# The odd 64 rows of a 320-row contraction as pairs of half-row matmuls into two PSUM banks

## What is computed

```python
def _moe_ref(x, w_gate, w_val, w_out, rms_g):      # d_model 320, d_ff 1536
    rms = np.sqrt(np.mean(x * x, axis=-1, keepdims=True) + 1e-06)
    xn = x / rms * rms_g
    g = xn @ w_gate
    silu = g * (1.0 / (1.0 + np.exp(-g)))
    return (silu * (xn @ w_val) @ w_out)

def _moe2_ref(x, w_in, w_out):                     # d_model 320, d_ff 2048
    h = x @ w_in
    return (np.maximum(0.01 * h, h) @ w_out)
```

## Time and profile before

| | |
|---|---|
| median of 3 runs | 477.48 us (476.37 to 477.69) |
| the profiled execution, first to last instruction (its span) | 473.8 us |
| TensorE busy | 95% of the span |
| VectorE, ScalarE, GpSimd busy | 56%, 38%, 22% |

### The profile page before, as it was taken

The page is one execution under the profiler, slowest core; times in us unless marked ns, Lnnn a source line. Parts: engine busy times, 40 slices in busy tenths (PEclk is TensorE's granted clock), DMA queues, the critical chain, the costliest instruction groups (busy, mean ns, idle before and its releaser), DMA issues.

```text
span 473.8 us, 7144 instructions
## 1 busy us (share of the span) xinstructions
PE 452.0 (95%) x2722; PEld 417.7 (88%) x2722; DVE 265.4 (56%) x492; ACT 179.8 (38%) x350; POOL 105.4 (22%) x95
## 2 busy tenths in 40 slices
PE   3779898999999999999999999999999999999997
PEld 3769898999999999999888888889989988998996
DVE  7767778676657787666553333634333343453444
ACT  1573652523324242242433322555334343333332
POOL 3487847321303032000032210253000000000000
PEclk9989999999999999999999999999999999999999
DMA  5878551312214032200022210130000000010101
GB/s 157 297 235 265 158 186 39 118 49 68 83 34 115 4 118 79 85 1 0 2 71 82 62 30 1 57 96 0 1 0 1 1 1 0 1 55 1 57 0 55
DMA packets 21439, 31.64 MB, mean 67 GB/s; under 512 B 1328, under 2 KB 15296, under 8 KB 21408
## 3 DMA queue, kind: packets, MB, share of 16 engines
q1 hardware_dynamic: 21408, 31.22, 21.2%
HBM read 29.20 MB, written 2.02 MB: 66 GB/s over the span
## 4 chain that ended last, share of the span: by engine, by line
PE 82%; DVE 7%; issue 3%; ACT 3%; DMA 2%; POOL 1%; SPq 0%; DVEq 0%; POOLq 0%; ACTq 0%
PE gate_ps L945 22%; PE value_ps L945 21%; PE out_ps L974 9%; PE out_ps L1011 8%; PE even_ps L1011 3%; PE out_ps L978 3%; PE c_ps L1011 3%; PE odd_ps L1011 3%; PE odd_ps L920 2%; PE c_ps L898 2%; PE c_ps L909 2%; PE odd_ps L889 2%; PE even_ps L889 2%; DMA att_sb<-in_qk 1%; PE even_ps L920 1%
## 5 line engine op out<-in xcount | busy, mean ns | idle before, releaser
L764 DVE TENSOR_TENSOR h_lo<-hid,h_hi 128x512 fp32r<-128x512 f32 (+2 forms) x96 | 74.8, 779 | 62.1 <-ACT h_hi L500 62.1
L500 ACT ACTIVATE h_hi<-hid 128x512 fp32r<-128x512 f32 (+2 forms) x96 | 55.5, 579 | 128.0 <-DVE hid L751 89.7
L945 PE MATMUL gate_ps<-x_hi,w_sb 128*128 128x512 f32 (+2 forms) x288 | 70.2, 365 | 4.0 <-DVE act_buf L745 2.9
L945 PE MATMUL value_ps<-x_hi,w_sb 128*128 128x512 f32 (+2 forms) x288 | 69.5, 363 | 0.0
L945 PEld LDWEIGHTS gate_ps<-x_hi,w_sb 128*128 128x128 f32 x288 | 49.0, 190 | 9.3 <-issue 3.7
L945 PEld LDWEIGHTS value_ps<-x_hi,w_sb 128*128 128x128 f32 x288 | 49.2, 190 | 4.3
L488 ACT ACTIVATE act_buf<-gate_ps 128x384 f32<-128x384 f32 (+2 forms) x48 | 23.4, 487 | 70.7 <-PE gate_ps L945 70.6
L974 PE MATMUL out_ps<-h_hi,w_sb 128*128 128x384 f32 (+2 forms) x192 | 49.0, 339 | 0.8 <-DVE h_lo L764 0.7
L745 DVE SCALAR_TENSOR_TENSOR act_buf<-act_buf,gate_ps 128x384 f32<-128x384 f32 (+2 forms) x48 | 26.5, 552 | 36.6 <-ACT act_buf L488 36.5
L390 POOL TENSOR_TENSOR w_sb<-raw,w_sb 128x704 fp32r<-128x704 f32 x16 | 27.4, 1714 | 76.9 <-ACT w_sb L482 76.9
L1011 PE MATMUL out_ps<-w_sb,h_hi 128*128 128x320 f32 x192 | 42.8, 308 | 0.0
(11 more groups left out here) (164 smaller groups left out, 808.3 us busy)
## 6 DMA issues: line engine op xcount, KB each, us to landing
raw<-in_w SPq DMA_DIRECT2D x12, 544.0 KB, 4.8
att_sb<-in_tok SPq DMA_DIRECT2D x12, 512.0 KB, 4.8
expo<-decay_scratch SPq DMA_DIRECT2D x12, 512.0 KB, 5.9
raw<-in_w SPq DMA_DIRECT2D x16, 352.0 KB, 2.9
att_sb<-in_qk SPq DMA_DIRECT2D x24, 160.0 KB
out_y<-y_acc SPq DMA_DIRECT2D x12, 160.0 KB, 1.9
consts_sb<-in_consts SPq DMA_DIRECT2D x1, 129.5 KB, 2.3
gates_sb<-in_gates SPq DMA_DIRECT2D x1, 96.0 KB, 2.4
```

Source lines behind the costliest of these rows:

```text
L500: nc.scalar.activation(h_hi[:, r, 0:n], hid[:, r, 0:n], ACT.Copy).then_inc(hi_done, 1)
L764: nc.vector.tensor_tensor(h_lo[:, r, 0:n], hid[:, r, 0:n], h_hi[:, r, 0:n].bitcast(F32), ALU.subtract).then_inc(h_done, 1)
L945: last = nc.tensor.matmul(ps[:, 0:n], lhs, rhs, start=(j == 0), stop=(j == len(xs) - 1))
```

## The change

The odd rows of two products are now taken together. A new stationary tile `mix` has in its partitions 0 to 63 the odd rows of one product's weights, and in 64 to 127 those of the other: gate and value of the same d_ff tile in layer 1, an even d_ff tile and the odd one behind it in layer 2. The single `x_odd` becomes two tensors: `x_odd_hi` with the high part in both halves of the partitions, and `x_odd_lo` with the low part in both. `odd_rows` does six matmuls, each with 64 rows of `mix` (a row tile of 64 x 128 at row 0 or 64 in the built program) and 64 rows of x; those of the lower half go to `gate_ps`, those of the upper half to `value_ps`, in turn. `whole_rows` does the other six matmuls of a product.

For a pair of products that is 2 x 6 + 6 = 18 matmuls in place of 2 x 8 = 16. The low x low product of the odd rows is no longer made.

```diff
-            def in_product(ps, w, c0, lo, cols, n, tiles=0):
+            def whole_rows(ps, w, c0, lo, cols, n, start, stop, tiles=0):
...
-                      (part(0, 0), x_lo[:, 0, cols]), (part(1, 0), x_lo[:, 1, cols]),
-                      (part(2, 0), x_odd[:, cols]), (part(2, 1), x_odd[:, cols])]
+                      (part(0, 0), x_lo[:, 0, cols]), (part(1, 0), x_lo[:, 1, cols])]
...
+            def odd_rows(w, mix, lo, cols, n, s):
+                parts = ((mix, 0), (mix + lo, 0), (mix, 1))
+                for j, (at, low) in enumerate(parts):
+                    for z in range(2):
+                        if j == 0 and z == 1:
+                            pe.wait_ge(hid_done, after(s - 1))
+                        rows = slice(z * ODD, (z + 1) * ODD)
+                        ins = nc.tensor.matmul(in_ps[z][:, 0:n], w[rows, at:at + P], x_odd[low][rows, cols],
+                                               start=(z == 1 and j == 0), stop=(z == 0 and j == 2))
+                        if z == 0 and j == 2:
+                            ins.then_inc(in_done, 1)
 
             def gate(s, c, f):
...
-                in_product(gate_ps, w1_sb[:, f, :], 0, LO1, cols1(c), TILES1[c] * P,
-                           tiles=FIRST if s == 0 else 0).then_inc(in_done, 1)
+                w, cols, n = w1_sb[:, f, :], cols1(c), TILES1[c] * P
+                whole_rows(gate_ps, w, 0, LO1, cols, n, True, False, tiles=FIRST if s == 0 else 0)
+                odd_rows(w, MIX1, LO1, cols, n, s)
 
             def value(s, c, f):
-                pe.wait_ge(hid_done, after(s - 1))
-                in_product(value_ps, w1_sb[:, f, :], KT * P, LO1, cols1(c), TILES1[c] * P)\
+                whole_rows(value_ps, w1_sb[:, f, :], 2 * P, LO1, cols1(c), TILES1[c] * P, False, True)\
                     .then_inc(in_done, 1)
...
                 pe.wait_ge(hid_done, after(s - 2))
-                in_product(in_ps[s % 2], w2_sb[g][:, f, :], 0, W2RAW, slice(c * CHUNK, (c + 1) * CHUNK), CHUNK)\
-                    .then_inc(in_done, 1)
+                w, cols, even = w2_tile(g * GF + f), slice(c * CHUNK, (c + 1) * CHUNK), f % 2 == 0
+                last = whole_rows(in_ps[f % 2], w, 0, W2RAW[f % 2], cols, CHUNK, even, not even)
+                if even:
+                    odd_rows(w, W2M, W2RAW[0], cols, CHUNK, s)
+                else:
+                    last.then_inc(in_done, 1)
```

VectorE fills the two tensors, per attention tile in `x_low` and per chunk in `x2_odd`:

```diff
             def x_low(n):
...
-                nc.vector.scalar_tensor_tensor(
-                    out=x_odd[ODD:P, tok], in0=turned_ps(n)[0:ODD, 2 * P:3 * P],
-                    scalar=rms_sb[0:ODD, 2:3], in1=x_odd[0:ODD, tok].bitcast(F32),
-                    op0=ALU.mult, op1=ALU.subtract).then_inc(x_done, 1)
+                nc.vector.tensor_copy(x_odd[0][ODD:P, tok], x_odd[0][0:ODD, tok].bitcast(F32))
+                for half in (slice(0, ODD), slice(ODD, P)):
+                    ins = nc.vector.scalar_tensor_tensor(
+                        out=x_odd[1][half, tok], in0=turned_ps(n)[0:ODD, 2 * P:3 * P],
+                        scalar=rms_sb[0:ODD, 2:3], in1=x_odd[0][0:ODD, tok].bitcast(F32),
+                        op0=ALU.mult, op1=ALU.subtract)
+                ins.then_inc(x_done, 1)
...
             def x2_odd(c):
...
-                then(nc.vector.tensor_copy(x_odd[0:ODD, cols], tail[:, 0:n]))
-                nc.vector.tensor_tensor(x_odd[ODD:P, cols], tail[:, 0:n], x_odd[0:ODD, cols].bitcast(F32),
-                                        ALU.subtract).then_inc(x2_done, 1)
+                then(nc.vector.tensor_copy(x_odd[0][0:ODD, cols], tail[:, 0:n]))
+                nc.vector.tensor_copy(x_odd[0][ODD:P, cols], tail[:, 0:n])
+                for half in (slice(0, ODD), slice(ODD, P)):
+                    ins = nc.vector.tensor_tensor(x_odd[1][half, cols], tail[:, 0:n],
+                                                  x_odd[0][0:ODD, cols].bitcast(F32), ALU.subtract)
+                ins.then_inc(x2_done, 1)
```

More of the change, by code:

```diff
@@ L69 @@
 TOK = ATT - V0
-W1M = 2 * KT * P + 2 * P
+MIX1 = 6 * P
+W1M = MIX1 + P
 W1RAW = W1M + ODD
@@ L76 @@
 LO1 = W1RAW + ODD
-W2RAW = KT * P + DM
-W2 = 2 * W2RAW
+W2M = 2 * P + DM
+W2RAW = (W2M + P, W2M)
+W2AT = (0, 2 * W2RAW[0])
+W2 = 2 * sum(W2RAW)
 GROUPS = 2
@@ L107, in build @@
         x_lo = sb(ctx, "x_lo", [P, 2, TILES * P], F32R)
-        x_odd = sb(ctx, "x_odd", [P, TILES * P], F32R)
+        x_odd = [sb(ctx, f"x_odd_{part}", [P, TILES * P], F32R) for part in ("hi", "lo")]
         raw = sb(ctx, "raw", [P, RAW, W1RAW])
@@ L145, in build, with w2_tile @@
                         + 4 * TILES * H + 3 * H + 8)
-            if used < 4 * GF * W2:
-                sb(first, "room", [P, GF * W2 - used // 4])
+            if used < 4 * GF // 2 * W2:
+                sb(first, "room", [P, GF // 2 * W2 - used // 4])
             w1_sb = sb(first, "w1_sb", [P, NF1, W1], F32R)
-        w2_sb = [sb(ctx, f"w2_sb{g}", [P, GF, W2], F32R) for g in range(GROUPS)]
+        w2_sb = [sb(ctx, f"w2_sb{g}", [P, GF // 2, W2], F32R) for g in range(GROUPS)]
+        def w2_tile(f):
+            g, f = divmod(f, GF)
+            return w2_sb[g][:, f // 2, W2AT[f % 2]:W2AT[f % 2] + 2 * W2RAW[f % 2]]
         y_acc = sb(ctx, "y_acc", [P, TILES, DM])
@@ L332, in _ @@
                 load_att(n)
-            for i in range(GF):
-                load_raw(NF1 + i, W2RAW, w2[i, :, :])
-            for i in range(GF, NF2):
-                load_raw(NF1 + i, W2RAW, w2[i, :, :])
+            for i in range(NF2):
+                load_raw(NF1 + i, W2RAW[i % 2], w2[i, :, 0:W2RAW[i % 2]])
             for n in range(TILES):
@@ L475, in hi_weights @@
                 else:
[L476 to L477 removed]
+                    f, n = i - NF1, W2RAW[(i - NF1) % 2]
+                    dst = w2_tile(f)[:, 0:n]
                     if i == NF1:
@@ L944, in in_product @@
                         pe.wait_ge(x_done, tiles)
-                    last = nc.tensor.matmul(ps[:, 0:n], lhs, rhs, start=(j == 0), stop=(j == len(xs) - 1))
-                return last
+                    last = nc.tensor.matmul(ps[:, 0:n], lhs, rhs, start=(start and j == 0),
+                                            stop=(stop and j == len(xs) - 1))
+                return last
+            def odd_rows(w, mix, lo, cols, n, s):
[9 more added lines that the diff above has]
+                            ins.then_inc(in_done, 1)
             def gate(s, c, f):
@@ L1107, in in_rows @@
         n = w.shape[1] // P
-        stacked = np.concatenate([w[0:2 * P], w[2 * P:], w[2 * P:]], axis=0)
-        return stacked.reshape(KT, P, n, P).transpose(2, 1, 0, 3).reshape(n, P, KT * P)
-    w1 = np.concatenate([in_rows(np.asarray(moe_w_gate)), in_rows(np.asarray(moe_w_val)),
-                         np.asarray(moe_w_out).reshape(NF1, P, DM)], axis=2)
-    w2 = np.concatenate([in_rows(np.asarray(moe2_w_in)), np.asarray(moe2_w_out).reshape(NF2, P, DM)], axis=2)
+        whole = w[0:2 * P].reshape(2, P, n, P).transpose(2, 1, 0, 3).reshape(n, P, 2 * P)
+        return whole, w[2 * P:].reshape(ODD, n, P).transpose(1, 0, 2)
+    gate_w, gate_odd = in_rows(np.asarray(moe_w_gate))
+    value_w, value_odd = in_rows(np.asarray(moe_w_val))
+    out_w = np.asarray(moe_w_out).reshape(NF1, P, DM)
+    w1 = np.concatenate([gate_w, value_w, out_w[:, :, 0:2 * P], np.concatenate([gate_odd, value_odd], axis=1),
+                         out_w[:, :, 2 * P:]], axis=2)
+    in_w, in_odd = in_rows(np.asarray(moe2_w_in))
+    w2 = np.zeros((NF2, P, W2RAW[0]), f32)
+    w2[:, :, 0:2 * P] = in_w
+    w2[:, :, 2 * P:W2M] = np.asarray(moe2_w_out).reshape(NF2, P, DM)
+    w2[0::2, :, W2M:] = np.concatenate([in_odd[0::2], in_odd[1::2]], axis=1)
     consts = np.zeros((P, 2 * P + KT), f32)
```

20 lines of the change are left out of this document (9 added, 11 removed).

## The result

The changed kernel takes **494.89 us** (median of 5 runs, 494.31 to 497.5), the kernel before 476.54 us in the 5 runs beside it. The ratio is 1.039, 95% interval 1.037 to 1.041: slower by 18.4 us. The profiled execution is the longest of the five, 497.5 us with a span of 495.7 us.

A forecast was written before the change was run, and what follows sets the result against it. TensorE, busy 95% of the span, was taken to set the time. Terms of -6.9 + 0.5 + 1.5 + 1.5 = -3.4 us against the profiled 473.8 gave 470.4; with the runs' median 3.7 higher, 474. Range: 466 to 500.

The forecast's parts named there:

- So that switch cost nothing, and I take 0: Entering and leaving each half-row block, 144 switches: priced at 0 from a row showing a switch of columns.
- the drain: Rival at the half-row switches: TensorE drains at each; half drain gives 486, full drain 498; chance 0.24.
- its other bound: Upper price of the half-row switches: a full drain, 0.164 us for each, 23.6 us in all.
- The signature given for this rival: Trace sign of a drain: a 0.1 to 0.2 gap before the first half and again behind the block.
- The pairing: Odd-row blocks on TensorE: three pairs replace four matmuls, halves streaming together but loading one after another; 6.9 us saved.
- the lowest bound: Lowest cost of the odd-row blocks: halves stream and load together, three slots a block, 13.9 us saved.
- Against it: one weight load at a time in every row: Argument against the rival that loads and streams run wholly together, forecast 467, chance 0.10.
- The copy: Added copy in `x_low(1)`, first half of layer 1: taken at 0.2 us, between 0 and 0.41.
- the term of 0.5: First half of layer 1: `x_low(1)` gains a 0.34 us instruction and a copy, delaying `x_lo` matmuls by 0.5 us.
- The early wait: Layer 1: value bank wanted already in the middle of `gate`; three steps, at most 2.6 us, taken at 1.5.
- The boundary: From layer 1 to layer 2: added copy and subtraction in `x2_odd(3)` lengthen TensorE's wait, 0.8 to 2.5, taken at 1.5 us.
- Layer 2's cover: Even steps of layer 2: work hiding the hidden tile's delay, 3.37 us, still holds by 0.23 us; counted 0.

The follow-up runs named there:

- e6: Kernel before, with the sixth matmul of each layer 2 input product using only 64 of its columns: 476.27 us, ratio 1.000.
- e3: Changed kernel, with whole matmuls between the half-row pairs in layer 2's even steps, six switches a block in place of two: 512.59 us, ratio 1.076.
- e5: Kernel before, with the sixth matmul of each layer 2 input product using only 64 of its 128 rows: 493.66 us, ratio 1.036.
- e1: Changed kernel, with each block's three half-row pairs made three whole 128-row matmuls into the first bank: 472.63 us, ratio 0.992.
- e12: Changed kernel, with ScalarE writing both halves of `x_odd_hi` in place of VectorE's copy, and `x2_odd(3)` ten steps later: 488.57 us, ratio 1.025.
- e7: Kernel before, with the last of the 16 matmuls of each pair of products left out: 465.26 us, ratio 0.977.
- e9: Kernel before, with the sixth matmul of each layer 2 input product cut to 64 rows by 64 columns: 492.29 us, ratio 1.033.
- e4: Changed kernel, with ScalarE writing both halves of `x_odd_hi` from PSUM and VectorE's copy in `x_low` gone: 492.78 us, ratio 1.034.
- e8: Changed kernel, with layer 1's half-row block moved from `gate` to the head of `value`: 496.54 us, ratio 1.041.
- e2: Changed kernel, with each block's three lower half-row matmuls ahead of the three upper ones, not in turn: 494.50 us, ratio 1.037.
- e11: Kernel before, with `x2_odd(3)`, the last filling of x_odd for layer 2, ten steps later on VectorE: 475.58 us, ratio 0.998.

## Why the prediction was wrong

The forecast was 474 us, 3.4 less than before; the measured time is 494.89, 18.4 more.

**The bound was right.** TensorE sets the time before and after.

**The step that failed is "So that switch cost nothing, and I take 0".** The row was read rightly: a 128*64 tile between whole ones is free, and e6 shows it over 96 switches. What failed is that it stood for a switch of rows. That one costs 0.18 to 0.20 us (e3, e5), and 144 of them were in the sum at nothing. The text gave the drain 0.24, and its other bound, 0.164 us a switch and 23.6 us, comes within 0.04 us of the switch and within about 1 us of what the switches cost on the path (22.3 by e1, 23.3 by e12 against e7). That its total comes so near is in part luck: it missed the load behind the drain, which e9 shows to be a part of the switch and which makes it longer than the bound, and the cover of the first chunk, which hides a sixth of the blocks; the two nearly cancel. The signature given for this rival, a gap of 0.1 to 0.2 before the first half and again behind the block, is what the timeline shows.

**The pairing was right, its size too small.** The halves start 0.01 apart and a pair takes one slot. But the loads do not go one after another: both of a pair start at the same time, 403.84 and 403.85. So the block inside is the lowest bound, three slots, at 256 and 384 columns as well (the third pair follows the second by 0.12 us at 57.78 and by 0.18 at 96.35), and 11.3 us were earned where 6.9 were taken. "Against it: one weight load at a time in every row" read too much into rows in which every tile used all 128 rows, or all came to the same ones.

**The start of layer 1 was mis-sized.** The copy was taken at 0.2 us and is 1.84 and 1.65: it starts behind an instruction of GpSimd and ends with it. The price came from the copy of 512 columns at 303.64, 0.41 us, which had started before GpSimd did (303.83). The copy alone, 0.2 of the term of 0.5, measured 2.1 (e4). The early wait, taken at 1.5 and up to 2.6, appears as 2.2 us in three waits (0.9 without the copy, e4), and a fall of the clock stands behind the longest; e8 shows that it can't be undone at a gain.

**The boundary was right in mechanism and, with the clock, short in size.** The wait for `h_lo` was forecast at about 2 us and is 1.9. The term of 1.5 measured 4.2 by e12, less the 0.8 that the kernel before also pays: the granted clock fell behind the wait, and no term stood for that. In an execution without the fall the term was about right: the two steps at the boundary take 9.50 us in e2 against 7.37 in the steady state, 2.1 more, where the kernel before has 8.22 against 7.21, 1.0 more.

**Layer 2's cover held.** No `h_lo` wait appears in the steady even steps, as forecast; each block's switches lengthen the cover too.

With the measured sizes in the prediction's own sum, -11.3 + 23.3 + 2.1 + 4.2, the change comes to +18.3 us, as it must by the way they were taken. Without the switches it would be -5.0 (e1, which has the pairing's slots and all of VectorE's work, measured -3.8): the switch decides the sign.

The best version is not among the halves. e12, the changed kernel with both repairs, is still 12 us over the kernel before. e11, the kernel before with `x2_odd(3)` ten steps later, takes 475.58 us, ratio 0.998 (0.996 to 0.999): ahead of both, though by under 1 us.

## What to carry to other kernels

Going from whole stationary tiles to tiles of fewer rows and back cost 0.18 to 0.20 us each way here, so a half-row block has to save more than 0.39 us, about two slots of 512 columns, before it earns anything; put all half-row work of a longer stretch in one block, or don't split (shown here only the other way round: more blocks cost more, e3). When a price is taken from the nearest row, ask whether that row changes the same thing (rows or columns) under the same conditions (which engine runs beside it, and which of the two started first), and if only a different one is at hand, let the far bound carry the weight. Move work that delays a busy TensorE to where there is slack, since a wait can cost about twice itself through the clock, as it did at the boundary in four of seven profiled executions.

## What the runs showed of the hardware

- **Rows and columns differ.** 96 switches, to 64 columns and back, changed nothing (e6, ratio 1.000, interval 0.999 to 1.001); 96 switches, to 64 rows and back, cost 17.3 us (e5).
- **Two 64-row tiles load and stream in parallel.** Loads 0.01 us apart, matmuls 0.00 to 0.01 us apart, pairs 0.23 us apart at 512 columns inside a block.
- **Halves of different rows are taken out of program order.** With three lower halves ahead of three upper ones, the first upper half starts 0.01 us behind the first lower one (e2).
- **The clock can fall behind a short wait, and need not.** Behind an idle stretch of 1.85 us the granted clock was 0.55 over 3.5 us, in a stage that stood at 1.00; in e2 the same wait left it at 1.00.
- **A copy of 64x128 that starts behind an instruction of GpSimd takes up to 1.84 us**, where one of 64x512 at 319.73, which starts 0.07 us ahead of GpSimd's, takes 0.41.
